# An attention, mixture-of-experts and rational-layer kernel: the first expert slot's rows formed by one-hot products, and a reordered hand-over to the dense block

## The reference

```python
mask = q_bucket[:, :, :, None] == k_bucket[:, :, None, :]
scores = np.where(mask, scale * np.matmul(q, k.transpose(0, 1, 3, 2)), -1000000000.0)
x = softmax(scores) @ v                      # 2 x 8 heads x 768 x 64 -> x: 1536 x 512
...
noisy = x @ w_gate + np.log1p(np.exp(x @ w_noise)) * noise
top2 = np.argpartition(-noisy, 2, axis=1)[:, :2]
for e in range(8):                           # w1: 512 x 1024, w2: 1024 x 512 per expert
    for k in range(2):
        mask = top2[:, k] == e
        h = np.maximum(x[mask] @ w1[e], 0.0)
        out[mask] += top2_w[mask, k, None] * (h @ w2[e])
...
h = out @ w_in                               # 512 x 2048
g = (a[0] + a[1]*h + a[2]*h**2 + a[3]*h**3) / (1 + abs(b[0])*abs(h) + abs(b[1])*h**2 + 1e-6)
return g @ w_out                             # 2048 x 512
```

## Time and profile before

| | |
|---|---|
| median of 3 runs | 968.96 us (968.41 to 969.49) |
| profiled execution | 965.89 us, of it the span 963.8 us |
| PE busy | 913.5 us, 95% of the span |
| DVE / ACT / POOL busy | 585.0 (61%) / 497.5 (52%) / 454.0 (47%) |
| granted PE clock, mean | 0.986 |
| the chain that ended last | PE 72%, DVE 10%, DMA 6%, issue 4%, POOL 3%, ACT 2% |
| attention / slots / dense block | 0 to about 283, 302 to 671, 682 to 964 us |

### The profile page before, as it was taken

How to read it: one execution, slowest core, us unless ns; L and a number is a source line. 1 busy time by engine, 2 the same in 40 slices (tenths; PEclk the granted TensorE clock), 3 DMA queues, 4 the chain that set the end, 5 groups by cost and what they waited for, 6 DMA issues and landing times.

```text
span 963.8 us, 17970 instructions
## 1 busy us (share of the span) xinstructions
PE 913.5 (95%) x5571; PEld 789.8 (82%) x5572; DVE 585.0 (61%) x1236; ACT 497.5 (52%) x889; POOL 454.0 (47%) x363
## 2 busy tenths in 40 slices
PE   5999999999964999999999999999799999999998
PEld 4888788888853888888888888888789999999997
DVE  7888888889775222222222222222689877777775
ACT  3877678778741222222222222222567777777775
POOL 5633353335444636545645455613677563553221
PEclk9999999999996999999999999999999999999999
DMA  7874355353339768977877688723811110110000
GB/s 186 201 226 123 103 141 134 93 140 78 121 136 280 220 198 268 295 216 240 269 233 224 211 239 282 264 87 107 263 39 62 56 35 11 54 44 0 34 1 33
DMA packets 85445, 143.25 MB, mean 149 GB/s; under 512 B 12562, under 2 KB 45074, under 8 KB 84882
## 3 DMA queue, kind: packets, MB, share of 16 engines
q1 hardware_dynamic: 44192, 72.06, 25.7%
q0 software_dynamic: 19328, 54.53, 17.8%
q10 hardware_dynamic: 21874, 16.00, 5.9%
HBM read 122.90 MB, written 19.66 MB: 148 GB/s over the span
## 4 chain that ended last, share of the span: by engine, by line
PE 72%; DVE 10%; DMA 6%; issue 4%; POOL 3%; ACT 2%; SPq 1%; DVEq 0%; ACTq 0%; POOLq 0%
PE ps_s L1187 18%; PE ps_o L1213 16%; PE ps_s L1271 13%; PE ps_t L1257 7%; DVE mx L1380 4%; DMA q_in<-in_q 4%; PE ps_s L1257 3%; PE ps_m L1257 3%; PE ps_s L1198 3%; PE ps_t L1070 3%; PE ps_o L1083 2%; PE ps_s L1061 1%; PE ps_s L1062 1%; DVE tile_t L1357 1%; DVE km L1373 1%
## 5 line engine op out<-in xcount | busy, mean ns | idle before, releaser
L596 POOL TENSOR_TENSOR w_r<-raw,w_r 128x1024 f32 (+1 forms) x72 | 172.1, 2403 | 107.7 <-DMA raw<-in_moe_w 46.9
L1187 PE MATMUL ps_s<-w_r,xT 128*128 x744 | 178.6, 396 | 14.8 <-DVE xT L1602 14.7
L1187 PEld LDWEIGHTS ps_s<-w_r,xT 128*128 128x128 f32 x744 | 138.4, 189 | 42.9 <-issue 15.1
L1213 PE MATMUL ps_o<-w_r,hT 128*128 x720 | 168.6, 390 | 0.0
L1213 PEld LDWEIGHTS ps_o<-w_r,hT 128*128 128x128 f32 x720 | 135.0, 188 | 27.9
L1271 PE MATMUL ps_s<-w_r,g_r 128*128 128x512 f32 x576 | 145.5, 398 | 4.5 <-DVE g_r L1699 4.5
L1612 DVE COPY y_sb<-ps_o 128x512 f32<-128x512 f32 x30 | 20.7, 691 | 196.0 <-PE ps_o L1213 196.0
L1271 PEld LDWEIGHTS ps_s<-w_r,g_r 128*128 128x128 f32 x576 | 107.6, 190 | 25.4 <-issue 4.6
L752 POOL TENSOR_TENSOR m<-q,g_r 128x384 f32<-128x384 f32 x64 | 66.0, 1031 | 110.8 <-DVE g_r L1687 110.6
L906 ACT ACTIVATE hT<-ps_s 128x1024 fp32r<-128x1024 f32 x30 | 30.8, 1027 | 154.9 <-DVE y_sb L1612 121.7
L821 ACT ACTIVATE prob<-ps_s,nb,sc 128x768 f32<-128x768 f32 x96 | 95.2, 992 | 21.1 <-DVE nb L1385 20.6
(11 more groups left out here) (260 smaller groups left out, 1505.4 us busy)
## 6 DMA issues: line engine op xcount, KB each, us to landing
w_r<-in_moe_w POOLq DMA_DIRECT2D x32, 1024.0 KB, 8.5
raw<-in_moe_w SPq DMA_DIRECT2D x56, 512.0 KB, 3.9
q_in<-in_q SPq DMA_DIRECT2D x56, 176.0 KB, 3.6
k_in<-in_k SPq DMA_DIRECT2D x56, 176.0 KB, 4.5
y_slots<-y_sb ACTq DMA_DIRECT2D x31, 256.0 KB, 4.7
xg<-x_slots ACTq DMA_DIRECT2D x120, 64.0 KB, 3.3
raw<-in_moe_w SPq DMA_DIRECT2D x16, 256.0 KB, 3.3
raw<-in_moe_w_in SPq DMA_DIRECT2D x8, 512.0 KB, 5.1
```

The source lines that it names most:

```text
L596: pool.tensor_tensor(of_chunk(buf, 1, n), raw[:, par, :], of_chunk(buf, 0, n).bitcast(F), ALU.subtract).then_inc(split_done, 1)
L1187: mm = pe.matmul(ps_s[0][:, o * 512:o * 512 + 512], xT[:, par, part, c * P:c * P + P], w_r[:, buf, wpart, col:col + 512], start=(c == 0 an ...
L1213: mm = pe.matmul(y_bank(i), hT_of(i)[:, half, c * P:c * P + P], w_r[:, buf, whalf, col:col + DM], start=(c == 0 and half == 0 and whalf == 0),
```

## The change

Two changes are made together.

**The first slot.** Slot 0 always gets rows 128 to 255 of `x_slots`, the first 128 rows of expert 0's region, whatever the counts are; the number of tiles of expert 0 is made at least one, and its count at least 256 where the row of its further slots is bounded. At the start SP clears these rows in DRAM (`first_zeroed`). The scatters of group 0 are due one step earlier, and after them SP loads the 128 rows as they then are into `x0_rows`; POOL waits for this load before the scatters of group 1 (they may write to the same rows). The share of tiles 6 to 11 is summed in PSUM by six fp32 products on PE (`first_rows`) with 0/1 matrices that DVE makes from `pos_f` (`first_places`). DVE adds the two into `x0_sum`, PE turns it by four transposes, and ACT and DVE round and split it as before. The route chain has the sum of x0 in its middle and the split of slot 0 at its end. All 24 scatters remain. The exponential of the routing weights on ACT and the late row table on POOL move behind other waits. Only slot 1 is still gathered right after the scatters.

**The hand-over.** In each slot ACT issues the store of y directly after the hT copy and no longer after relu and the next gather. At the end of the slots DVE copies y of slot 29 after the first combine, and y of slot 30 after the others. `first_sum` of slot None uses the transpose form of the product. POOL issues the second half of the `w_out` transfer before its splits 2 and 3, and no longer after them.

```diff
--- before.py
+++ after.py
...
+LOADED = GROUPS[0][1]
...
+    first_row = small("first_row", [P, P], F)
...
+    first_oh = at("first_oh", 176 * KB + 512, [P, NT - LOADED, P], F)
+    x0_rows = at("x0_rows", 132 * KB, [P, DM], F)
+    x0_sum = at("x0_sum", 134 * KB, [P, DM], F)
...
+                if first:
+                    sp.dma_start(x_slots[P:2 * P, :], zeros[:]).then_inc(first_zeroed, 16)
...
+            sp.wait_ge(tile_split, (PAIRS - 1) * NTILES)
+            sp.wait_ge(scattered, 16 * 2 * LOADED)
+            for g in range(Q):
+                quad = slice(g * (P // Q), (g + 1) * (P // Q))
+                sp.dma_start(x0_rows[quad, :], x_slots[P + g * (P // Q):P + (g + 1) * (P // Q), :]).then_inc(xg_loaded[0], 16)
...
-            first_rows = [sp.value_load(slot_row[0:1, i:i + 1], min_val=0, max_val=E * REGION - P) for i in range(2)]
+            row = sp.value_load(slot_row[0:1, 1:2], min_val=0, max_val=E * REGION - P)
-            for i in range(2):
-                for g in range(1, Q, 2):
-                    quad_load(sp, i, first_rows[i], g)
+            for g in range(1, Q, 2):
+                quad_load(sp, 1, row, g)
+            sp.wait_ge(x_turned, 1)
...
+            pool.memset(region_t[:, 0, 0:1], P - 1.0).then_inc(route_const, 1)
+            pool.iota(first_row[:], [[1, P]], base=P, channel_multiplier=0,
+                      allow_small_or_imprecise_dtypes=True).then_inc(route_const, 1)
...
+                if g == 0:
+                    pool.wait_ge(first_zeroed, 16)
+                if g == 1:
+                    pool.wait_ge(xg_loaded[0], 16 * Q)
-                        pool.wait_ge(x_done, (PAIRS - 1) * T + i - 2)
+                        pool.wait_ge(x_done, (PAIRS - 1) * T + i - 3)
+            for loaded in xg_loaded:
+                pool.wait_ge(loaded, 16 * Q)
-            for loaded in xg_loaded:
-                pool.wait_ge(loaded, 16 * Q)
...
-            split_some(E + 1, 1, range(CHUNKS // 2))
+            split_some(E + 1, 1, range(2))
+            split_some(E + 1, 1, range(2, CHUNKS // 2))
...
-            act.wait_ge(diff_ready, 1)
-            act.activation(wts[:, 1, :], diff[:], ACT.Exp).then_inc(act_route, 1)
...
+            xT_hi_out(0, 0)
-            first_rows = [slot_rows(i) for i in range(2)]
+            row = slot_rows(1)
+            act.wait_ge(diff_ready, 1)
+            act.activation(wts[:, 1, :], diff[:], ACT.Exp).then_inc(act_route, 1)
-            for i in range(2):
-                load_xg(i, i, first_rows[i], range(0, Q, 2))
-            xT_hi_out(0, 0)
+            load_xg(1, 1, row, range(0, Q, 2))
...
+                if y:
+                    store_y(i - 2, par)
...
-                if y:
-                    store_y(i - 2, par)
...
-                    pe.wait_ge(route_const, 12)
+                    pe.wait_ge(route_const, 14)
...
+            def first_rows(i):
+                pe.wait_ge(first_made, i - LOADED + 1)
+                mm = pe.matmul(ps_t[:, 0:DM], first_oh[:, i - LOADED, :], x_sb[:, i].rearrange("p g c j -> p (g c j)"),
+                               start=(i == LOADED), stop=(i == NT - 1))
+                if i == NT - 1:
+                    mm.then_inc(first_summed, 1)
...
+                    for i in range(LOADED, LOADED + 3):
+                        first_rows(i)
+                    for i in range(LOADED + 3, NT):
+                        first_rows(i)
+                    pe.wait_ge(x0_summed, 1)
+                    for c in range(DC):
+                        mm = pe.transpose(ps_m[:, c * P:c * P + P], x0_sum[:, c * P:c * P + P], ident[:])
+                    mm.then_inc(x_turned, 1)
...
-                        mm = pe.matmul(first_bank[j][:, cols], x2_first[:, j, cols], ident[:],
+                        mm = pe.matmul(first_bank[j][:, cols], x2_first[:, j, cols], ident[:], is_transpose=True,
...
-                    dve.wait_ge(route_const, 12)
+                    dve.wait_ge(route_const, 14)
...
+            def first_places(*tiles):
+                for i in tiles:
+                    dve.wait_ge(pos_ready, [g for g, (t0, t1) in enumerate(GROUPS) if t0 <= i < t1][0] + 1)
+                link(*[dve.tensor_scalar(first_oh[:, i - LOADED, :], first_row[:], pos_f[:, 0, i:i + 1], None, ALU.is_equal) for i in tiles])
+                for i in tiles:
+                    dve.scalar_tensor_tensor(out=first_oh[:, i - LOADED, :], in0=first_row[:], scalar=pos_f[:, 1, i:i + 1],
+                                             in1=first_oh[:, i - LOADED, :], op0=ALU.is_equal, op1=ALU.add).then_inc(first_made, 1)
...
+                    first_places(6, 7)
+                    first_places(8)
+                    first_places(9)
+                    first_places(10, 11)
...
-            link(dve.tensor_reduce(tiles_e[:], cmp_sb[:], AX.X, ALU.add))
+            link(dve.tensor_reduce(tiles_e[:], cmp_sb[:], AX.X, ALU.add),
+                 dve.tensor_scalar(counts[:, 0:1], counts[:, 0:1], 2.0 * P, None, ALU.max))
...
+            dve.wait_ge(first_summed, 1)
+            dve.wait_ge(xg_loaded[0], 16 * Q)
+            dve.tensor_tensor(x0_sum[:].rearrange("p (c g j) -> p g c j", g=Q, j=P // Q),
+                              ps_t[:, 0:DM].rearrange("p (g c j) -> p g c j", g=Q, j=P // Q),
+                              x0_rows[:].rearrange("p (g c j) -> p g c j", g=Q, j=P // Q), ALU.add).then_inc(x0_summed, 1)
...
+            def split_x(i, par):
+                dve.wait_ge(xT_hi, i + 1)
+                dve.tensor_tensor(xT[:, par, 1, :], ps_m[:, :], xT[:, par, 0, :].bitcast(F), ALU.subtract).then_inc(xT_ready, 1)
+            split_x(0, 0)
...
-            def split_x(i, par):
-                dve.wait_ge(xT_hi, i + 1)
-                dve.tensor_tensor(xT[:, par, 1, :], ps_m[:, :], xT[:, par, 0, :].bitcast(F), ALU.subtract).then_inc(xT_ready, 1)
...
-            for i in range(2):
-                turn_x(i, 0, i)
-                split_x(i, i)
+            turn_x(1, 0, 1)
+            split_x(1, 1)
...
-            for j in range(TB):
+            combine(0)
+            copy_y(SLOTS - 2, (SLOTS - 2) // 2, (SLOTS - 2) % 2)
+            for j in range(1, TB):
-            copy_y(SLOTS - 2, (SLOTS - 2) // 2, (SLOTS - 2) % 2)
```

More of the change, by code:

```diff
@@ L260, in fused_kernel @@
     scattered = sem("scattered")
+    first_zeroed = sem("first_zeroed")
+    first_made = sem("first_made")
+    first_summed = sem("first_summed")
+    x0_summed = sem("x0_summed")
     rows_ready = sem("rows_ready")
```

## The result

The changed kernel takes 961.65 us (median of 9 runs, 957.84 to 964.65) where the kernel before takes 968.30 (9 runs, 965.51 to 969.49): ratio 0.9935, 95% interval 0.9917 to 0.9953. It is faster by 6.65 us (4.6 to 8.0 by the interval). The time lies in the forecast range of 955 to 963, 2.5 us above the forecast of 959.2; the gain of 9.7 that was forecast lies outside the measured interval.

What follows compares the result with a forecast made beforehand. PE, busy 95% of the span, was taken as the bound, so only its pauses could give time. Front 6.2 plus tail 3.5 made 9.7 us, subtracted from the 968.96 median: 959.3, taken as 959.2; range 955 to 963.

Steps and rivals of the forecast that it cites:

- The signs: Profile after: slot 0's product about 6 us earlier, slot 1 near 305, scatters unmoved, joint's pauses reduced or gone.
- The front (6.2): Attention's end to slot 0: first product at 295.7 instead of 301.87, 6.2 us earlier, with DVE becoming the bound.
- The tail (3.5): Joint between slots and dense block: 2.3 + 0.55 + 0.65 = 3.5 us gained.
- The sums as transposes and the vanished wait: Joint: first sums take 1.3 instead of 2.9, and a 0.65 us wait goes; L1257 starts 2.3 us earlier.
- The dense block's way to the first g: Joint, pause before L1271: POOL's earlier product gives 0.55 us more, bounds 0 and 1.4.
- The stall of the y gather: Joint: earlier weight transfer frees the y gather, removing PE's wait at 704.81; 0.65 us gained.
- the earlier due times at no cost: Attention: group 0's scatters, due earlier, let x0 rows land by 276.1, 2.4 us of cover before group 1; no price.
- Rival 2: Slot 0's product: clock still high because the six products fill the pause; 1.5 us, 957.7; chance 0.30 with rival 1.
- Rival 1: Joint: clock holds through the shorter pause before L1271; 1.5 us, 957.7; chance 0.30 with rival 2.
- Rival 6: Scatters: late x0 load gates all twelve; gain eaten if it lands 15 us late, 971 at 17; chance 0.03.
- Rivals 4 and 5: Joint: transposes no faster, 960.8 (0.20 shared with rival 3); edit: slot 0 early, slot 1 late as now, 965.4 (0.05).
- rival 3: Front: new wait from low-clock products, one-hots at upper price or late x0 loads; 961; chance 0.20 shared with transposes case.

Runs made afterwards that it cites:

- spacing in their place: Changed kernel with group 0's scatters in threes, each behind one value product, and group 1's last scatter likewise: 955.28 us, ratio 0.9891.
- spacing alone: Kernel before with only group 0's scatters in threes behind value products and group 1's fourth behind the last one: 964.34 us, ratio 0.9959.
- the clock kept at slot 0: Changed kernel with scatters in threes, plus two readerless PE products before the x0 transposes and two behind them: 951.65 us, ratio 0.9851.
- before with fills: Kernel before with all twelve group 0 scatters due at once, POOL filling a scratch tile seven times after each three: 966.14 us, ratio 0.9990.
- more bytes: Kernel before with scatters in threes, plus twelve plain transfers of the scatters' size on SP's queue: 964.36 us, ratio 0.9962.
- the front alone: Kernel before with the first-slot part and its earlier due time, without the hand-over edits at the joint: 963.90 us, ratio 0.9980.
- the experiment with the due time of before: Changed kernel with group 0's scatters due as in the kernel before, one step later: 958.33 us, ratio 0.9918.

## Why the prediction was right, and where it was not

**The signs.** The time fell into the range, but the profile did not show all that the prediction asked of it. By its own words it would be wrong "if the scatters move". Slot 0's product starts at 303.85, 2 us later than before and not 6 earlier, slot 1's at 313.4 instead of near 305, and the scatters end at 301.44 instead of 293.60. All of this is the 7.8 us inside the attention; counted from the attention's end, the signs of the front came as forecast.

**The front (6.2) was right.** 6.03 in the profile after, and 12.1 us from the last `x_sb` copy to slot 0 in all six profiles that have the edit with early rows. Its parts: one-hots for tiles 10 and 11 take 296.13 to 297.26, 1.13 instead of 0.87 (within its bounds 0.4 and 1.6); the sum of product and rows 0.69 (0.70); split and issue 0.61 + 0.66 (0.70 + 0.45). Scatters did not move against the attention's end, slot 1 was not bound: it starts 9.55 us behind slot 0, where it was 9.44. The fp32 products hide behind DVE; two together take 1.88 us in the timeline, 0.94 each, where I charged 0.86.

**The tail (3.5) was right in sum, with single terms off.** The sums as transposes and the vanished wait gave 2.27 (2.3). The twelve transposes last from 674.37 to 675.68, where L1327 begins: 1.31 (1.3), 0.11 each. The price that the Trainium skill gives, "TensorE: Matmul & The Clock Gate", section "Part 4: PE-mode transpose", about 275 ns for one in a kernel, would by my estimate make 3.3 of it; the trace has 40% of that. (The eight in 0.88 us, too, are 40% of that price and not a third, as the prediction says.) The dense block's way to the first g brought 1.50 where I took 0.55: the upper bound, 1.4, was the better reading, since POOL's product came earlier, 6.90 us behind the first product of the dense block (689.61 - 682.71) where it was 8.71 (690.74 - 682.03), and the first g came earlier with it. The stall of the y gather gave 0.48, not 0.65. And a term was missing: six gathers of y now run where the last slot's `hT` copy stands, and PE waits 0.77 there. That these belong together is only argued, by the copy's start at 666.21, 0.9 us behind the end of the product that it waits for (665.29), beside an unbroken row of six gathers that ends at 666.41. The wait is there in five of the seven profiles that have the hand-over edits (0.73 to 1.48) and in none without them.

**The step that failed: the earlier due times at no cost.** The forecast used them ("With the earlier due times, the last scatter of group 0 is the one that now starts at 268.59") for the loads of x0 alone, and put no price on the row of six that they make. Moved alone they cost 6.0 us on the kernel before (3.8 to 8.1). On the changed one, spacing in their place, which also breaks group 1's row, brings 4.4 (0.9937 against 0.9891). My rule, to charge every instruction of a moved step on each queue, was kept for POOL's own queue and the loads. It did not ask what a longer unbroken row on POOL does to the others, and no row of the trace before shows it: there neither the two rows of four nor the row of eight held a signal.

**The base was not what its profile showed.** I subtracted terms read from one profiled execution without a hold from the median of executions of which the typical one has some: spacing alone takes 3 to 4 us off the kernel before. That the sum still came within 2.5 us is luck: two errors of opposite sign, the loss without a price and a base that was itself too slow. With both kernels spaced, the ratios differ by 0.0068, 6.6 us with an error of some 2.4, where the profiles' front and tail make 9.5; with the clock kept at slot 0 the difference is 10.4, less its 1.5: 8.9. So some 3 us of the spaced kernel's median are unexplained, hardly more than the error. Its executions outside the profiled one show a mean clock of 0.991 to 0.995 against 0.998 in it, so further low stretches are likely, but where they lie no trace shows.

**The rivals.** Rival 2 (clock high at slot 0) did not come by itself: in the pause the clock was still high (1.00 in the window 300 to 302), but it fell as the product began (0.68 and 0.50 in the two windows below), and the product took 7.35 as if it had been low before. With products placed in the 5 us ahead, it held. Rival 1 (clock holds at the joint) has the wrong condition: after pauses of 3.49 (before with fills) and 3.42 us (more bytes) the nine products took 2.29 and 2.32, after 3.49 in the front alone 3.77, and after a pause of 2.12 in the kernel after 3.79. The pause's length alone decides nothing there. Rival 6 has a real gate, by the experiment with the due time of before, where the x0 rows held group 1 back by 5.8 us; slot 0 came 2.5 later there, mostly by the late signals beside the merged row and not by the rows' landing, far from turning the sign. Rivals 4 and 5 did not occur. Of rival 3 the clock part shows in the same experiment: there the last three products (six instructions) took 4.54 us at the low level, and the sum came 0.44 us late.

## What to carry to other kernels

When transfers that an engine issues one by one are made due earlier, count how many then stand in one unbroken row, and look whether others' signals arrive beside that row; beside the attention three with a pause of 1 us cost next to nothing here, six cost 4 us at once and more through the clock. Beside the routing eight cost nothing, so look at each place. Take the price of such an edit by itself: one digit moved alone told in one run what the whole change hid. And read a term as lost only after cutting both profiles at the same landmarks, since here the net of 1.5 us between two spans was made of -6.0, -3.5 and +7.8.

## What the hardware showed that I had not expected

- ACT waited 3.9 to 4.1 us for PE's completion signal behind a finished product when POOL had issued six indirect transfers in a row beside the attention (four profiles; the signal came 1.03 to 1.08 us after the row's end each time), 1.2 to 2.4 us beside some rows of four and not at all beside others, and 4.0 us and again beside a row of twelve, where the first signal came 1.07 us after the sixth scatter's end. Beside rows of three signals were late by at most 0.7 us; beside two scatters, in two profiles, by 1.3.
- Beside a row of eight, during the routing, signals were not late (0.03 us at its end); beside a row of twelve there DVE's own signal was, by 1.0 us. In the stall with the row of twelve no semaphore but those of DMA changed between 253.88 and 257.81.
- Nearly twice the bytes on the DMA engines (366 GB/s, share 1.00) did not do it, and no transfer of instructions stands in the stall of the kernel after (256 to 261). What path the signals and POOL's issuing share stays open, and so does why a row of four is held in one execution and not in the next.
- In the kernel after, the granted clock was still at its high level (2.4 GHz) while PE stood ahead of slot 0, and fell to the low one (1.2 GHz) only within the product that begins at 303.85. Its windows:

```profile
300.00:302.00 2.00, 0.66 (x4) 0.42 (x4) 1.90 (x6) 0.60 (x1) 1.14 (x2) 1.00 0.39 150
304.00:306.00 2.00, 2.00 (x7) 1.60 (x8) 1.83 (x6) 0.00 (x0) 0.00 (x0) 0.68 0.44 123
306.00:308.00 2.00, 2.00 (x7) 1.52 (x6) 1.76 (x10) 0.00 (x0) 1.04 (x2) 0.50 0.97 258
```

- Start-up differs from execution to execution: the first scatter of the changed kernel starts at 252.17 us in one profile and at 250.74 in another, and over all profiles between 248.6 and 252.2.
